# Stacking v with the solved vectors z in one tile, moving solver steps and sums of squares to the vector engine, and reordering every engine's program

## The reference

```python
for t in range(S):
    y[:, :, t] = einsum('bhd,bhde->bhe', rt, state)
    Sa = einsum('bhde,bhe->bhd', state, at)
    state = state * wt[:, :, None, :] - einsum('bhd,bhe->bhde', Sa, bt)
    state = state + einsum('bhd,bhe->bhde', vt, kt)
x = y.transpose(0, 2, 1, 3).reshape(B * S, H * D)
h = x @ w_in;  g = where(h >= 1, h, where(h <= -1, 0, (h + 1) ** 2 / 4));  x = g @ w_out
h = maximum(maximum(x @ w1, x @ w2), x @ w3);  out = h @ w_out2
```

## Time and profile before

| | us |
|---|---|
| median of 3 runs | 1079.31 (1077.81 to 1084.52) |
| the profiled execution | 1085.12 |
| its span, from the first to the last instruction | 1083.4 |
| start of y of the first, the last group | 99.3, 453.1 |
| the first product of `dense` | 457.65 |

### The profile page before, as it was taken

One profiled execution on the slowest core, in us unless ns is written; L12 is line 12 of the kernel. 1 busy time (PEld: TensorE's weight loads), 2 busy tenths in 40 slices (PEclk: granted clock), 3 DMA queues, 4 the chain that ended last, 5 costly groups with the idle time before them and its releaser, 6 DMA issues.

```text
span 1083.4 us, 31839 instructions
## 1 busy us (share of the span) xinstructions
PE 980.2 (90%) x13194; PEld 826.0 (76%) x13194; DVE 467.5 (43%) x642; ACT 384.4 (35%) x719; POOL 451.4 (42%) x669
## 2 busy tenths in 40 slices
PE   5678887898988778699999999999999999999998
PEld 4557676787777667576788888878887888788887
DVE  7636454554644233199324323333333233324331
ACT  1114344444444344366313322332233233313321
POOL 3789393764929477033213312331232133223311
PEclk9668899998999888899999999999999999999999
DMA  5854654655654453155100000010001000100000
GB/s 92 126 106 75 116 99 92 117 96 116 103 118 90 91 99 67 44 169 151 30 1 24 12 19 25 0 29 0 25 0 29 0 24 0 29 0 24 1 1 25
DMA packets 242923, 61.40 MB, mean 57 GB/s; under 512 B 223728, under 2 KB 238832, under 8 KB 242800
## 3 DMA queue, kind: packets, MB, share of 16 engines
q1 hardware_dynamic: 149872, 45.19, 18.8%
q10 hardware_dynamic: 92928, 14.43, 8.4%
HBM read 44.89 MB, written 14.68 MB: 55 GB/s over the span
## 4 chain that ended last, share of the span: by engine, by line
issue 26%; PE 17%; POOL 10%; DVE 3%; ACT 1%; DMA 0%; POOLq 0%; DVEq 0%; ACTq 0%; SPq 0%
POOL hid_lo L1344 10%; PE ring L1157 7%; PE acc L1157 5%; PE ring L1167 3%; PE ring L1199 2%; DVE sq L1400 1%; DVE clip L1394 1%; PE acc L1221 1%; DVE wmax_lo L1370 1%; DMA raw<-in_moe_w_dram 0%; ACT hid_hi L1282 0%; ACT sq L1306 0%; DVE wout_lo L1362 0%; POOLq L35 0%; DVE win_lo L1370 0%
## 5 line engine op out<-in xcount | busy, mean ns | idle before, releaser
L1344 POOL TENSOR_TENSOR hid_lo<-sq,hid_hi 128x512 fp32r<-128x512 f32 x132 | 173.3, 1313 | 452.2 <-ACT hid_hi L1282 452.2
L433 POOL TENSOR_TENSOR prod<-sysX 128x30 f32<-128x30 f32 (+14 forms) x210 | 111.1, 529 | 62.4 <-DMA sysX<-systems 48.3
L437 POOL TENSOR_TENSOR sysX<-sysX,prod 128x30 f32<-128x30 f32 (+14 forms) x210 | 117.0, 557 | 16.5
L1394 DVE TENSOR_SCALAR clip<-ring 128x512 f32<-128x512 f32 x96 | 66.2, 689 | 132.0 <-PE ring L1167 132.0
L1282 ACT CAST hid_hi<-sq 128x512 fp32r<-128x512 f32 x132 | 82.0, 622 | 92.2 <-DVE sq L1400 70.1
L1306 ACT ACTIVATE sq<-clip 128x512 f32<-128x512 f32 x96 | 60.7, 632 | 145.7 <-DVE clip L1394 143.8
L1400 DVE SCALAR_TENSOR_TENSOR sq<-clip,sq 128x512 f32<-128x512 f32 x96 | 67.3, 701 | 59.5 <-ACT sq L1306 59.5
L1157 PE MATMUL acc<-hid_hi,wout_hi 128*128 128x512 f32 x192 | 76.1, 396 | 8.0 <-POOL hid_lo L1344 7.9
L1157 PE MATMUL ring<-x_hi,win_hi 128*128 128x512 f32 x192 | 75.5, 393 | 3.3 <-PEq L903 3.3
L1425 DVE TENSOR_TENSOR sq<-ring,clip 128x512 f32<-128x512 f32 x36 | 24.9, 692 | 120.4 <-PE ring L1167 98.1
L1328 ACT COPY clip<-ring 128x512 f32<-128x512 f32 x36 | 21.1, 587 | 153.8 <-PE ring L1167 153.8
(11 more groups left out here) (170 smaller groups left out, 2161.8 us busy)
## 6 DMA issues: line engine op xcount, KB each, us to landing
nat_r<-in_r_dram SPq DMA_DIRECT2D x96, 40.0 KB
vrv<-in_v_dram SPq DMA_DIRECT2D x96, 40.0 KB
xT<-yT SPq DMA_DIRECT2D x96, 40.0 KB
out_dram<-res SPq DMA_DIRECT2D x24, 160.0 KB, 1.8
inverses_T<-sysX SPq DMA_DIRECT2D x7, 512.0 KB, 3.8
nat_w<-in_w_dram ACTq DMA_DIRECT2D x44, 80.0 KB, 3.1
nat_a<-in_a_dram ACTq DMA_DIRECT2D x44, 80.0 KB, 3.7
nat_b<-in_b_dram ACTq DMA_DIRECT2D x44, 80.0 KB
```

The lines of the kernel that those rows point to most:

```text
L433: g_.tensor_tensor(some, X[:, 0:j, j:j + 1].to_broadcast([P, j, rest]), X[:, j:j + 1, j + 1:BLK].to_broadcast([P, j, rest]), ALU.mult)\
L437: g_.tensor_tensor(X[:, 0:j, j + 1:BLK], X[:, 0:j, j + 1:BLK], some, ALU.add)\
L1344: nc.gpsimd.tensor_tensor(hid[at % HB][1][:, :], sq[at % 2][:, :], f32(hid[at % HB][0][:, :]), ALU.subtract)\
L1394: nc.vector.tensor_scalar(clip[f % 2][:, :], ring[(f + 2) % 4][:, :], -1.0, None, ALU.max).then_inc(clipped, 1)
```

## The change

It touches `attention` and one wait in `dense`.

- v and z share a tile `vz` with 128 partitions: for batch j, the rows of j hold v and the other 64 rows hold z. The tile `kb` has kn in the rows of j and bn in the others. So one product over 128 partitions takes the place of two over 64 (`xy`), one set of transposes (`vz`) that of v's and z's, one set of scores (`rr`) that of rv and rz. The scaling of k on POOL writes its result for both halves (128x16x40 in place of 128x8x40). Two DVE copies (`bk`) bring bn into kb.
- z is negated in two ACT instructions of 64 partitions; k's transposes become 8 of 64 rows; dn's products become transposes.
- `ys` is cut in two (`ys`, `yt`), with other work between them.
- Both sums of squares (840 and 512 columns) go from ACT to DVE.
- The first 19 of the 30 solver steps of unit 1 (groups 2 to 5) go from POOL to DVE, at the end of its START.
- The first loads of k, r and v no longer come in one block behind the first unit's load; they have places in START and the loop.
- PE leaves out waits that an earlier wait already covers (`need`).
- All tables are new, solver steps begin at turn first-4 for units 2 to 5 (and first-5 for unit 6) and not first-3, `inverse` and `solved` stand one group further ahead, and a table FINISH takes over at turn 21.

```diff
-        vrv = ring("vrv", NATS["v"], [P, 2, 2, HP, W])
-        zrz = sb("zrz", [P, 2, 2, HP, W])
+        vz = ring("vz", NATS["v"], [P, 2, 2, 2, HP, W])
...
-        kn = ring("kn", LATE, [P, HP, 2, W])
+        kb = ring("kb", LATE, [P, 2, HP, 2, W])
...
-            "SP": [("load r0", 2), ("solved", 0), ("inverse", 0), ("dense", -1), ("system", 7), ("load v1", 3),
-                   ("unit", 7), ("load r1", 3), ("load v0", 3), ("y", -1)],
+            "SP": [("load r0", 3), ("load r1", 3), ("solved", 1), ("load v0", 1), ("load v1", 1), ("inverse", 1),
+                   ("system", 8), ("dense", -1), ("y", -1), ("unit", 8)],
...
-        SOLVE_FROM, SOLVE_AT = 3, 0
+        START_LEN, FINISH_FROM = 20, 21
+        VECTOR_STEPS, VECTOR_FROM = 19, 9
+        FIRST_STEP = {0: 0, 1: 38}
+        SOLVE_FROM, SOLVE_AT = [3, 3, 4, 4, 4, 4, 5], 2
...
-                if u == 0:
-                    for at in range(4):
-                        for n in ("k", "r", "v"):
-                            if at < NATS[n]:
-                                for j in range(2):
-                                    load(sp, n, j, 0)(at)
...
+            def kn_(g):
...
+                twice = [x.unsqueeze(1).to_broadcast([P, 2, H, D])
+                         for x in (natural("k", g), recip(g).rearrange("t (h e) -> t h e", h=H))]
+                g_.tensor_tensor(kb[g % LATE][:, :, :, :, :].rearrange("t j p s e -> t j (p s) e")[:, :, :, 0:D],
+                                 *twice, ALU.mult).then_inc(kn_made, 1)
...
+            def need(signal, value):
+
+                if value > waited.get(signal, 0):
+                    pe.wait_ge(signal, value)
+                    waited[signal] = value
...
+            def rr(g):
+                need(out["vz"], g + 1)
+                need(out["r"], g + 1)
+                ps = begin("rr", g)
+                for j in range(2):
+                    for m in range(HP):
+                        for i in range(2):
+                            at = (j * HP + m) * CH
+                            last = nc.tensor.matmul(ps[:, i, at:at + CH], vzT[rows(i), j, m, :],
+                                                    rT[g % LATE][rows(i), m, j, :], start=True, stop=True)
...
             def xy(g):
-                pe.wait_ge(out["rz"], g + 1)
-                pe.wait_ge(out["rv"], g + 1)
-                pe.wait_ge(out["z"], g + 1)
-                pe.wait_ge(kn_made, g + 1)
-                pe.wait_ge(done["ys"], 2 * (g + 1))
+                need(out["rr"], g + 1)
+                need(bk_made, 2 * (g + 1))
+                need(done["yt"], g + 1)
...
-                    for left, right in ((kn[g % LATE], vrv[g % NATS["v"]]), (bn[g % EARLY], zrz)):
+                    for j in range(2):
                         for s in range(2):
-                            for j in range(2):
-                                last = nc.tensor.matmul(ps[rows(s), j, p * P:(p + 1) * P], left[rows(j), p, s, :],
-                                                        right[rows(j), :, s, p, :],
-                                                        start=False, stop=True, skip_group_check=True)
+                            last = nc.tensor.matmul(ps[rows(s), j, p * P:(p + 1) * P], kb[g % LATE][:, j, p, s, :],
+                                                    vz[g % NATS["v"]][:, :, j, s, p, :],
+                                                    start=False, stop=True, skip_group_check=True)
...
+            def squares(x, column, g, checked):
+                ge(dve, totalled, g - 3)
+                nc.vector.scalar_tensor_tensor(junk[column][:, :], x, 1.0, x, ALU.mult, ALU.mult,
+                                               accum_out=sums[g % 4][:, column:column + 1]).then_inc(checked, 1)
```

More of the change, by code:

```diff
@@ L199, in attention @@
         for n, g in sequence("PE"):
-            if n not in OPENS:
+            if n not in OPENS and n not in MORE:
                 before[n, g] = last.get(BANK[n])
@@ new lines, in b_, with k_ @@
+                transposed("b", g, bn[g % EARLY])
+            def k_(g):
+                need(kn_made, g + 1)
+                ps = begin("k", g)
+                for p in range(HP):
+                    for j in range(2):
+                        last = nc.tensor.transpose(ps[:, j, p * CH:(p + 1) * CH],
+                                                   kb[g % LATE][rows(j), j, p, :, :].rearrange("t s e -> t (s e)"),
+                                                   ident[rows(j), rows(j)])
+                last.then_inc(done["k"], 1)
@@ new lines, in vz_ @@
+            def vz_(g):
+                need(out["z"], 2 * (g + 1))
+                ps = begin("vz", g)
+                for j in range(2):
+                    for m in range(HP):
+                        s, q = divmod(m, 2)
+                        src = vz[g % NATS["v"]][:, 0, j, s, 2 * q:2 * q + 2, :]
+                        last = nc.tensor.transpose(ps[:, j, m * P:(m + 1) * P], src.rearrange("t i e -> t (i e)"),
+                                                   ident[:, :])
+                last.then_inc(done["vz"], 1)
@@ L580, in gs @@
             def gs(g):
[L581 removed]
+                need(out["a"], g + 1)
                 if g < 2:
[L583 to L585 removed]
+                    need(zeroed, ZEROED)
+                need(stT_made, g - 1)
+                need(done["g"], g + 1)
                 ps = bank_of["g"]
@@ L617, in st_, with state_by_r @@
                 last.then_inc(done["st"], 1)
+            def state_by_r(g, turn, done_):
+                ps = bank_of["ys"]
+                for q in range(HP // 2):
+                    for i in range(2):
+                        for s in range(2):
+                            p, j = 2 * q + i, i ^ turn
+                            last = nc.tensor.matmul(ps[rows(s), j, p * P + CH:(p + 1) * P],
+                                                    st[g % 2][rows(i), j, q, s, :],
+                                                    rT[g % LATE][rows(i), 2 * s + q, j, :],
+                                                    start=turn == 0 and q == 0, stop=False, skip_group_check=True)
+                last.then_inc(done_, 1)
@@ L619, in ys @@
             def ys(g):
                 if g < 2:
-                    pe.wait_ge(zeroed, ZEROED)
-                ge(pe, out["st"], g - 1)
-                pe.wait_ge(out["r"], g + 1)
-                ps = begin("ys", g)
-                for turn in range(2):
-                    if turn == 1:
-                        pe.wait_ge(done["ys"], 2 * g + 1)
-                    for q in range(HP // 2):
-                        for i in range(2):
-                            for s in range(2):
-                                p, j = 2 * q + i, i ^ turn
-                                last = nc.tensor.matmul(ps[rows(s), j, p * P + CH:(p + 1) * P],
-                                                        st[g % 2][rows(i), j, q, s, :],
-                                                        rT[g % LATE][rows(i), 2 * s + q, j, :],
-                                                        start=turn == 0 and q == 0, stop=False, skip_group_check=True)
-                    last.then_inc(done["ys"], 1)
@@ L1391, in one_block @@
                     mine = list(split_pieces(f - 1)) if first else []
+                    if first and f == 0:
+                        dve.wait_ge(y_stored, 64 * NG)
                     ge(dve, h_done, n * T1 + f + 1)
```

292 lines of the change are left out of this document (151 added, 141 removed), and 34 rows, old and new, of tables (FINISH, ORDER, START).

## The result

The changed kernel takes **1108.2 us** (median of 4 runs, 1106.4 to 1109.0); the kernel before took 1079.0 beside it. The ratio is 1.026 (95% interval 1.023 to 1.029): 29 us slower, where 1038.5 and a range of 1016 to 1064 had been forecast. The profiled execution took 1108.5, its span is 1106.8 for 1083.4 before. So the two traces differ by 23 us and not by 29: the profiled execution of the kernel before lay 6 us above its median.

What follows compares the result with a forecast made beforehand. PE was taken as the bound ahead of dense, losing time to late inverses. Start +3, 15 turns -37.2, last 8 turns -6.6 sum to -40.8: 1044.3 from the profiled 1085.1, stated as 1038.5 us against the runs' median; range 1016 to 1064.

Steps and rivals of the forecast that it cites:

- The waits for inverses go: Full turns: DVE's 45 us of waits for inverses vanish; POOL, next late, takes 13.6 us a turn, under PE's 14.0.
- A whole turn of slack: Solver steps begin a turn earlier and inverses' stores and loads stand a turn ahead, giving those 45 us of waits slack.
- The sums of squares: On DVE, together 1.8 us; slowing of POOL by overlaps, sums and copies was taken as 1.6 us of its turn.
- the 15 turns: Turns from y of group 0 to y of group 15: 15 x 14.0 = 210 us for 247.2, -37.2 us.
- Rival 4: Shared DVE and POOL ports slow start (+28 us) and loop (POOL's turn 16.0): +21, 1100 us; chance 0.05.
- The scores: PE's turn: two sets (1.14 us) become one with weights twice as wide; between 0.57 and 2.06, taken 1.1, no gain.
- the 13.8 of the sum: PE's work in an ordinary turn: 14.43 + 0.15 - 0.15 + 0.05 - 0.7 = 13.8 us.
- The chain: From z's negation to masked scores within a turn: 3.3 us grows by 2.5; a leftover 0.2 makes the turn 14.0.
- the sign that was named for vzT: The forecast is wrong if PE waits for vzT or the masked scores by over 0.5 us a turn.
- Rival 3: Chain shows in full turns: ACT's transfers and 1024-column copy delay PE 1 us more, turn 15.0: 1056 us; chance 0.14.
- The start: Before the loop: 19 unit 1 solver steps on DVE put the first inverse at 88 for 85.06 us: +3 us.
- The last 8 turns: Turns after the work done ahead runs out: grown chain gives 12.5 us each, 100 for 106.6 us, -6.6 us.

Runs made afterwards that it cites:

- the one-input reads: Changed kernel with squares on ACT and, on DVE where the sums stood, unused maxima over the same 840 and 512 columns: 1087.4 us, ratio 1.0066.
- Three edits of the start: Eleven buffers, 64x64 scores, squares on ACT, k's scaling on DVE, plus: 9 DVE solver steps and early loads/store (1073.3); early loads/store alone (1062.9); 14 steps, early loads/store, SP reordered (1071.2).
- the second trace of the same loop: Kernel with eleven buffers, 64x64 scores and squares on ACT, plus kb copies and y ahead of dense's splits in FINISH on DVE: 1064.6 us, ratio 0.9876.

## Why the prediction was wrong

**The step that failed** is "The waits for inverses go", where it put POOL at 13.6 us a turn, "just under PE's", and so put the sums of squares and POOL's place in the chain at nothing. The runs showed three costs in its place: 22 us by the sums of squares on DVE, 12 by the scan that waits for POOL's stT, and, from another step, 15 by the scores. Each is what its edit gives back alone; together they give back 45, more than the 29 lost, since other parts of the change do gain.

- *A mean for a turn.* 38 us for a unit and 9.5 a group is a mean over 30 steps of 30 to 240 columns. POOL's program puts up to 13 steps between two stT, whatever their width: none in some turns, the widest 13 in others, which with kb and stT take 23.5 us. The number to be compared with PE's turn was this one.
- *"A whole turn of slack."* True of the inverses, whose wait fell from 45.0 to 3.0 us. But the scan went one group further ahead in a ring of the same ten buffers, and 13 steps stand where 11 stood, so it lost the turn of slack that it had towards stT. The prediction asked what was late next and named POOL, but did not follow who waits for POOL. Eleven buffers gave 12 us of it back, then the solve itself was next; SP's wait for it wasn't, by the run with SP's order changed.
- *The sums of squares.* Taken as 1.6 us of POOL's turn, with overlaps and copies, and set to nothing since PE's turn covered it. Undone alone they are 22 us, the largest part. In the trace POOL's instructions were stretched by some 11 us beside the sums in the 240 us from 110 (for each instruction its length less the shortest of its form, put down to the DVE instruction that overlaps it most), about 3 us for a unit's solve; beside the one-input reads it is 0.4. In the profiled runs 6.8 us of the gain are in the 15 turns and 11.1 in the last 8. That more is lost than the stretch itself I put down to the turns in which POOL is the bound and to PE's clock behind each idle stretch; that part is argued and not taken apart. Rival 4, slower by the shared ports, named the largest cause and came nearest with its 1100, but its 28 us sat in the start, which lost 8.9 for other reasons, so its number is in part luck. Its chance was 0.05.
- *The scores*, "between 0.57 and 2.06 I take 1.1": 1.94 measured, near the upper end, and 15 us of the kernel by the run with 64x64 scores. This is the term of the turn's sum that was mis-sized. The reason given for 1.1, half of dn's moving columns, does not hold: 61 ns per instruction for 64 columns, where dn had 64 ns for 128.
- *xy*, 2.0 taken: 1.89. *dn*, 0.88: 0.96. *k*, 0.55: 0.40. *The cut ys*, 0.9: 0.76. These were right: the 13.8 of the sum, plus the scores' 0.84, less 0.32 for these four, is 14.32, and the ordinary turn took 14.36. *The chain*: PE's waits for vzT sum to 5.2 us in 14 times and for the inverses' copies to 10.1 in 20, both below 0.5 a turn, the sign that was named for vzT. Rival 3 (the chain, a turn of 15.0) did not come: the ordinary turn is 14.36.
- *The start*, +3: +8.9. The first inverse came at 89.7 for the 88 forecast, so 19 steps were priced right (17.8 us of DVE's time for "14 to 18"). Missed was PE: it had nothing to do for 10 of 15 us and then went through most of its first turn at half clock. Three edits of the start gave y of group 0 at 104.7, 110.8 and 102.8, of which only the last is clear of the 104.4 to 111.4 that traces with the changed kernel's START show, and that by 1.6. What it would take to win it back stays open.
- *The last 8 turns*, -6.6: +13.1. The order in which FINISH puts y behind the splits for `dense` and three sums is 3.9 of it by the trace (7 by the time of the whole kernel); the sums as such are 11.1 (the two overlap). Without sums on DVE these turns take 108.6 us, and with eleven buffers and 64x64 scores besides 102.6, near the 100 forecast.
- With the three causes taken away the 15 turns take 220.4 (216.0 in the second trace of the same loop) and the forecast was 210. The 10 us between are three turns of 16.8 to 18.1; that POOL's solve is still their bound fits the run with k's scaling on DVE, in which they are gone.

Of the signs named in advance, three said it at once: turns above 15, xy and scores apart (2 and 1.94 in place of 2 and 1.1), and no clock at 1.0 (0.92). The mean of POOL's solver instructions (0.56 and 0.59, below the 0.65 named) did not: it was set for a full POOL, and one that is late now and then is enough. The 1108 lie outside every rival: "slower" had 0.06 in all.

## What to carry to other kernels

Count an engine's work between two instructions that others wait for, at its widest, not its mean in a turn. When a stage is moved one turn ahead in a ring, give the ring one more buffer, or look who reads the old contents last: here the missing one cost 12 us. And before work is moved to VectorE, look at whether it reads two operands from SBUF while GpSimd is near the critical path: 46 us of such work cost 22, 38 us of one-input reads cost 1.

## What the runs showed of the hardware

- 32 matmuls with 64 rows, 128 weight columns and 64 moving columns took 1.94 us (61 ns each); the same work in 64 matmuls of 64x64 took 1.1 (17 ns each). What is measured is the two times; that more of the products run side by side in the second form fits them, but no view here shows it.
- A GpSimd sum of 228 columns took 1.51 us beside a VectorE instruction with two SBUF inputs of 1.02 us, and 0.63 without it; beside a one-input read of the same 840 columns a sum of 220 columns took 0.61 us.
- A gap of 4.8 us on TensorE was followed by scores at 3.68 us for 1.94: the granted clock is 1.00 from 154 to 160 us, falls within the gap, and is 0.50 from 163 to 173, the lower level, 1.2 GHz. So a wait of 5 us cost 9 in that turn (24.1 for 15).
